# Fused attention, MLP and rotation kernel on one core: other steps for the attention stages, and layer norm's two scalings in steps of their own

## The reference

```python
# 1: attention, 8 heads of 64; each query sees its last n_local keys and the first n_global keys
scores = q @ k.T / sqrt(64) - slope[head] * dist
a = softmax(where(keep, scores, -1e9))
x = a @ v                                   # (2, 768, 512)
# 2: MLP
xn = (x - mean) / sqrt(var + 1e-6) * g_ln   # per token
x = x + relu(xn @ w_ch1) @ w_ch2            # 512 -> 2048 -> 512
# 3: rotation and token mixing
theta = x @ w_theta
u = x + w_tok_r @ (x * cos(theta)) + w_tok_i @ (x * sin(theta))
out = u + relu(u @ w_ch)
```

## Time and profile before

| | |
|---|---|
| time, median of 3 runs | 549.47 us (549.36 to 549.56) |
| profiled execution, its own time | 549.34 us |
| its span, first to last instruction | 547.5 us |
| PE busy | 537.8 us (98%) |
| DVE / ACT / POOL busy | 266.2 / 171.2 / 185.7 us |
| TensorE clock granted | 1.000, mean of the span |
| scores / attend / transposes of probabilities, PE | 26.1 / 25.6 / 23.4 us |
| masks (L428) on DVE, exps (L484) on ACT | 32.9 / 46.0 us |

### The profile page before, as it was taken

How to read it: one execution, slowest core, us unless ns; L and a number is a source line. 1 busy time by engine, 2 the same in 40 slices (tenths; PEclk the granted TensorE clock), 3 DMA queues, 4 the chain that set the end, 5 groups by cost and what they waited for, 6 DMA issues and landing times.

```text
span 547.5 us, 8685 instructions
## 1 busy us (share of the span) xinstructions
PE 537.8 (98%) x3376; PEld 482.0 (88%) x3376; DVE 266.2 (49%) x678; ACT 171.2 (31%) x438; POOL 185.7 (34%) x165
## 2 busy tenths in 40 slices
PE   8899999999999999999999999999999999999997
PEld 7788788788888888998889998888799999999997
DVE  7765655556547454222222322355865669307054
ACT  5564443444435332111111111265555422001010
POOL 6596000000000000398000410033499799362500
PEclk9999999999999999999999999999999999999999
DMA  7663243211221000033100110000022133341202
GB/s 227 199 221 90 83 146 113 74 56 45 87 65 45 1 1 2 0 135 101 73 1 0 54 34 1 0 1 1 1 57 63 55 86 88 115 116 62 83 21 95
DMA packets 24810, 36.95 MB, mean 67 GB/s; under 512 B 2240, under 2 KB 17600, under 8 KB 24768
## 3 DMA queue, kind: packets, MB, share of 16 engines
q1 hardware_dynamic: 24768, 36.38, 21.4%
HBM read 33.23 MB, written 3.15 MB: 66 GB/s over the span
## 4 chain that ended last, share of the span: by engine, by line
PE 81%; POOL 10%; DVE 4%; issue 3%; ACT 1%; DMA 0%; POOLq 0%; DVEq 0%; ACTq 0%
PE bank L882 13%; PE bank L865 13%; PE bank L1471 12%; PE bank L1087 12%; PE bank L1105 11%; PE bank L1489 6%; POOL trig L1232 4%; PE bank L535 4%; PE bank L505 3%; PE bank L520 3%; POOL ring_l L1215 3%; PE bank L1323 3%; POOL ring_h L1212 2%; POOL bias L412 1%; PE bank L803 1%
## 5 line engine op out<-in xcount | busy, mean ns | idle before, releaser
L865 PE MATMUL bank<-xnT,w1h 128*128 128x256 f32 x384 | 73.7, 291 | 1.3 <-DVE xnT L826 1.3
L865 PEld LDWEIGHTS bank<-xnT,w1h 128*128 128x128 f32 x384 | 59.7, 191 | 7.2 <-issue 5.0
L1087 PE MATMUL bank<-xnT,w1h 128*128 128x384 f32 x256 | 65.2, 335 | 0.0
L1471 PE MATMUL bank<-ring_h,z_hi 128*128 128x384 f32 x192 | 65.0, 338 | 0.1
L1471 PE MATMUL bank<-ring_h,z_lo 128*128 128x384 f32 x192 | 64.3, 335 | 0.0
L1471 PE MATMUL bank<-ring_l,z_hi 128*128 128x384 f32 x192 | 64.2, 335 | 0.0
L484 ACT ACTIVATE sp_buf<-sp_buf,row_max 128x256 f32<-128x256 f32 (+1 forms) x96 | 46.0, 481 | 42.3 <-DVE row_max L428 42.3
L795 POOL TENSOR_TENSOR rstd<-rtmp,minus_half 128x2 f32<-128x2 f32 x6 | 4.2, 697 | 154.6 <-DVE rtmp L766 154.6
L1232 POOL TENSOR_TENSOR trig<-x,trig 128x512 f32<-128x512 f32 x24 | 32.8, 1387 | 67.7 <-ACT trig L1279 67.7
L865 PE MATMUL bank<-xnT,w1l 128*128 128x256 f32 x192 | 54.3, 283 | 0.0
L1215 POOL TENSOR_TENSOR ring_l<-raw,ring_h 128x768 fp32r<-128x768 f32 x24 | 48.0, 2001 | 2.0
(11 more groups left out here) (124 smaller groups left out, 1124.9 us busy)
## 6 DMA issues: line engine op xcount, KB each, us to landing
raw<-wtokT SPq DMA_DIRECT2D x24, 384.0 KB, 3.2
raw<-w SPq DMA_DIRECT2D x8, 1024.0 KB, 5.7
v_sb<-vwin SPq DMA_DIRECT2D x16, 256.0 KB, 2.7
k_sb<-kcols SPq DMA_DIRECT2D x16, 200.0 KB, 3.3
q_sb<-qT SPq DMA_DIRECT2D x24, 128.0 KB, 2.8
outT<-out_sb SPq DMA_DIRECT2D x16, 192.0 KB, 1.8
v_sb<-vwin SPq DMA_DIRECT2D x8, 192.0 KB, 2.9
k_sb<-kcols SPq DMA_DIRECT2D x8, 136.0 KB, 2.8
```

Source lines behind the costliest of these rows:

```text
L865: last = nc.tensor.matmul(bank_of(n)[:, 0:AN], wt[q][:, d, f * P:(f + 1) * P], xnT[:, AT * c:AT * c + AT, low, d, :], start=(d == 0 and m ...
L1087: last = nc.tensor.matmul(h_bank[f % 2][:, 0:CN], wt[slot][:, d, fs], tokens(low, d), start=first, stop=(d == DC - 1 and wt is w1l))
L1471: last = nc.tensor.matmul(bank, zt[b][:, s, r, ds], wt[j % RING][:, r, :], start=(s == 0 and r == 0 and m == 0), stop=(s == TILES - 1 and ...
```

## The change

Three things are altered. The tables of the attention stages get other steps for blocks 8 to 23: attend of a block and scores of the next block now have one step in common, which puts them next to each other on PE (attend, then scores). The step of xT 0 to xT 3 goes from 19, 20, 20, 22 to 20, 20, 22, 22 in chunks 1 to 4 (chunk 0 keeps 21, 21, 22, 22). Layer norm's statistics of chunks 2 to 5 go two steps later (13 for 11), and in all chunks but the first `norm_scale` is cut into its two instructions, one and two steps behind `norm_newton` (before both were issued with it).

```diff
-            where = (21, 21, 22, 22) if c == 0 else (19, 20, 20, 22)
+            where = (21, 21, 22, 22) if c == 0 else (20, 20, 22, 22)
...
-        SCORES_AT = {place_at(k, (-12, -7, -2, 4)): k for k in range(8, BLOCKS)}
-        TRANSPOSE_AT = {place_at(k, (-7, -3, 2, 8)): k for k in range(8, BLOCKS)}
-        ATTEND_AT = {place_at(k, (-5, -2, 4, 10)): k for k in range(8, BLOCKS)}
-        BACK_AT = {place_at(k, (-4, -1, 5, 11)): k for k in range(8, BLOCKS)}
+        SCORES_AT = {place_at(k, (-12, -4, 0, 8)): k for k in range(8, BLOCKS)}
+        TRANSPOSE_AT = {place_at(k, (-7, -1, 5, 11)): k for k in range(8, BLOCKS)}
+        ATTEND_AT = {place_at(k, (-4, 0, 8, 12)): k for k in range(8, BLOCKS)}
+        BACK_AT = {place_at(k, (-3, 1, 9, 13)): k for k in range(8, BLOCKS)}
...
-        SECOND_EXPS_AT = {place_at(k, (-10, -5 if k == 9 else -6, -1, 6)): k for k in range(8, BLOCKS)}
+        SECOND_EXPS_AT = {place_at(k, (-10, -2, 3, 10)): k for k in range(8, BLOCKS)}
...
-        STATS_AT = {16: 1, **{place_at(k, (0, 0, 0, 11)): k // PAIRS for k in range(11, BLOCKS, PAIRS)}}
+        STATS_AT = {16: 1, **{place_at(k, (0, 0, 0, 13)): k // PAIRS for k in range(11, BLOCKS, PAIRS)}}
...
-        def norm_scale(dve, c):
+        def norm_scale(dve, c, us=range(AT)):
...
-            for u in range(AT):
+            for u in us:
...
-                    norm_scale(dve, STATS_AT[s - 2])
+                for u in range(AT):
+                    if s - 3 - u in STATS_AT:
+                        norm_scale(dve, STATS_AT[s - 3 - u], (u,))
```

## The result

| | before | after |
|---|---|---|
| median, runs in turn on the same chip | 549.56 us (549.32 to 549.89, 9 runs) | 548.18 us (547.91 to 548.47, 9 runs) |
| profiled execution, its span | 549.34, 547.5 us | 548.37, 546.6 us |
| ratio, 95% interval | | 0.9975 (0.9964 to 0.9985) |

The account below looks back on a forecast made before the run. PE was taken to bound the early MLP stretch (186.13 of 188.00 us busy). Terms -1.4 - 1.5 - 1.5 + 2.5 + 0.5 = -1.4 gave 547.9 from the profiled 549.34, so a 548.1 us median; range 546.3 to 549.5.

Parts of the forecast that it names:

- Seven more pairs: On PE, attend and the next scores become neighbours seven times, each saving 0.20 us of seams: 1.4 us less.
- Step 20, chunk 0: Attend and scores (2.3 us) between g9 and g10, with fewer DVE instructions before g9's low part, remove a 1.5 us stall.
- Step 20, chunks 1 to 3: Attend and scores cover 2.3 us against the 1.09 g9's low part needs: 3 x 0.5 = 1.5 us less.
- Step 22, the new wait: In chunks 0 to 4, g11 must wait until DVE takes g10 out: 5 x 0.5 = 2.5 us more.
- the subtraction of 0.41 from 0.93: At step 22, g11 could start 0.93 after g10's end; four transposes cover 0.41, leaving 0.5 us per chunk.
- The count of DVE's queue: From xT 0 and 1 in step 20, DVE could begin g10's way out at 3.68, needed at 3.58: 0.1 late.
- the rival of a late DVE: At step 22 DVE comes half a us late in four chunks, stall 1.0 there: +0.6, 550.1 us; chance 0.24.
- Steps 12 to 20, layer norm behind more masks: In chunks 1 to 3, DVE's chain makes attend at step 20 wait 0.15 three times: 0.5 us more.
- the adding up of recorded durations: From the scores of step 12, DVE's durations sum to 8.3 against PE's 8.05; 0.15 taken instead of 0.3 for overlap.
- DVE's chain ahead of attend decides: Step 20 of chunks 1 to 3, step 22 of chunks 0 to 3: masks paid in full, +2.7, 552.2 us; chance 0.08.
- there is no new wait: At step 22, g10 comes out under the transposes, so the 2.5 isn't paid: 545.6 us; chance 0.1.
- A sign of being wrong that came: The prediction would be wrong if masks on DVE start later than 1.2 us behind their scores.

Follow-up runs that it names:

- Experiment 1: Changed kernel with the scores of the third block of each chunk (blocks 10, 14, 18, 22) one step behind attend: 549.03 us, ratio to before 0.9994.
- experiment 2: Changed kernel with both layer norm scalings together again in the step of newton: 548.06 us, ratio to before 0.9977.
- Experiment 3: Kernel before with only the two scalings split into steps of their own, one and two behind newton: 549.17 us, ratio to before 0.9994.
- experiment 5: Changed kernel with transposes back and write_x of each chunk's first block at step 22 instead of 21: 547.01 us, ratio to before 0.9960.
- experiment 6: Changed kernel with xT 0 to xT 3 of chunks 1 to 4 at steps 19, 20, 20, 22 again: 547.63 us, ratio to before 0.9973.

## Why the prediction was right, and where it wasn't

- *Seven more pairs*: right in mechanism and size. Experiment 1 took four apart and paid 0.85 for the 0.8.
- *Step 20, chunk 0*: right, 1.58 for 1.5. The step named two reasons, cover and fewer instructions ahead of the low part; experiment 2 shows that the cover and the masks do it, and that the split, which I counted among them, adds at most 0.08. Experiment 3 shows that the split alone would have met ACT's queue. The low part is done 1.80 after g9's end and not 1.03, so 0.4 of the cover was left over, not 1.3.
- *Step 20, chunks 1 to 3*: right, 0.54 each for 0.5.
- *Step 22, the new wait*: the mechanism, the releaser and the distance are as forecast (0.95 for "about 0.95", in all five chunks), but the term was mis-sized: 0.61 each, 3.05 for 2.5. The step that failed is the subtraction of 0.41 from 0.93. Half of the miss, 0.05, is the cover: the 0.41 of the earlier trace rows has the seam between scores and transposes in it; here, behind output matmuls, four transposes cover 0.36. The rest is small: 0.95 for 0.93, a seam of 0.10 behind the wait where four transposes leave one of 0.08 anyway, and 0.52 rounded to 0.5. The count of DVE's queue came out 0.1 better than feared: from the start of xT 0 in chunk 3 DVE is free 3.57 later (3.68 in the count), and the turn of g10's way out comes after 3.69 (3.58 in the count). That leaves a margin of 0.12 in chunks 2 and 3, so the rival of a late DVE was close.
- *Steps 12 to 20, layer norm behind more masks*: the term was mis-sized, 0.0 for 0.5. DVE's chain from the start of the scores, predicted 8.3, is 7.99 in chunk 3 (162.89 to 170.88, rows below), and attend starts at 170.98, where it would have started unhindered. The failing step is the adding up of recorded durations: instructions of DVE behind each other start up to 0.1 before the end of the one in front, and I discounted that by half. The low part of g7 lengthens the way from `write_x` to the scalings by 0.20 (3.83 for 3.63) and not by 0.42, and the two scalings take 0.90 until the copy and not 1.01. The copy ends only 0.10 before attend starts, so the term is 0 by a thin margin.

```profile
162.89 1.14 PE L505 MATMUL bank<-k_sb,q_sb 64*128 64x256 f32 x8
164.07 0.42 DVE L428 CUSTOM_DVE_ANT_0 sp_buf<-bank,bias 128x256 f32<-128x256 f32 x1 [1.46 <-PE bank L505]
...
165.46 0.42 DVE L471 TENSOR_TENSOR x<-bank,inv 128x256 f32 x1
...
169.29 1.00 DVE L787 TENSOR_SCALAR xn<-x,mean_var,rstd 128x512 f32<-128x512 f32 x2
170.19 0.69 DVE L443 COPY probsT<-bank 128x512 f32<-128x512 f32 x1
```

- *The rivals.* That DVE comes half a us late at step 22 is refuted: g10's way out starts 0.20 behind PE in all chunks. That DVE's chain ahead of attend decides is refuted by the same rows; masks start 0.35 apart (four from 164.07 to 165.11, `write_x` at 165.46). That there is no new wait is refuted by the brackets at step 22.
- *A sign of being wrong that came.* The prediction calls itself wrong if masks start later than 1.2 behind their scores. After the scores of step 20 they start 2.63 to 2.84 behind in chunks 1 to 3, because the low parts of xT 0 and 1 stand ahead of them on DVE, as the count of DVE's queue at step 22 itself had them. The sign was too wide: elsewhere the masks start up to 1.22 behind, and PE waits for none of these.

The two errors, 0.55 too little at step 22 and 0.5 too much for layer norm, cancel by luck, so the total says less for the method than its closeness suggests. What the runs do confirm one by one are the pairs, both stalls at step 20 and the nature of the wait at step 22.

Not tried: a fourth shared bank for g10. By the turn rule it should remove the wait at step 22, but no run shows it.

## What to carry to other kernels

Price a matmul stage by the distance of starts around it, seams included: stages that use the array in another shape belong next to each other, here 0.20 us per pair. When banks go round in turns, moving a use of one shifts who waits for whom for all turns behind it; write out the turn three back before and after, and look at what its evacuation is queued behind. A fixed latency such as the evacuation of the last group is a place to put work, and filling it (experiment 5) gave another 0.95 to 1.2 us, where the whole change gave 1.4.

## What the hardware showed that I had not expected

- The first output matmul after a wait takes 0.33 to 0.34 until its successor instead of 0.23. That isn't the wait's alone: behind attend and scores it is 0.34 with no wait, behind transposes 0.31. Where hidden matmuls stand on both sides of a wait (experiment 6, g9 in chunk 4), the first one behind it takes 0.22 instead of 0.12. So a wait costs 0.10 more than its gap between matmuls of one kind, and 0.02 more behind transposes.
- DVE instructions in a row overlap: masks of 0.42 start 0.35 apart, scalings of 0.55 some 0.45 apart. The Trainium skill, VectorE: DVE Perf Modes, section on the DRAIN you can't avoid, makes an exception for a next instruction that isn't held, which the prediction left out. The section on two Vector instructions with no wait between them in the same page of the Trainium skill says, as a model, that an instruction is held when it starts in another quadrant (a group of 32 partitions) than the ones in front. All of these instructions take all 128 partitions, so none is held, and the rows agree.
- Where the early MLP starts differs between executions of nearly the same program by over 0.4 us (27.49 to 27.94 in the twelve traces), as much as a third of this change.
